# Turning the gathered rows of a mixture-of-experts stage on VectorE and a DMA queue instead of TensorE

## The chip, the cores and the metric

One core of one Trainium2 chip runs the whole program. The metric is the device time of one execution in microseconds (us); lower is better. The engines are TensorE (PE in the rows, its weight loads PEld), VectorE (DVE), ScalarE (ACT), GpSimd (POOL) and SyncE (SP), which here only issues DMAs.

## The reference, cut to what matters

Three stages follow one another: a linear-attention recurrence gives 3072 rows `x` of 384 numbers, a first network (a mixture of 8 experts) sends each row through one expert, and a dense second network follows.

```python
for e in range(E):                       # E = 8, D = 384, F = 1024
    mask = expert_idx == e
    h = np.maximum(x[mask] @ w1[e], 0.0)
    out[mask] = gate_w[mask, None] * (h @ w2[e])
...
h = x @ w_in                             # 3072 x 384 @ 384 x 2048
g = np.maximum(0.01 * h, h)
return (g @ w_out).astype(np.float32)
```

## The kernel before, in words

Each engine has its own instruction stream, and semaphores join them. Every fp32 product is made of three fp32r products (high x high, high x low, low x high parts), so each operand is split by ScalarE (the high part, a copy) and VectorE (the low part, a subtraction).

**The first network** works in 31 windows of 128 slots (`WINDOWS`), sorted by expert. A slot holds a row number, or none. For a window, which the code calls a block while it is ahead, the steps are these:

- POOL gathers its 128 rows from DRAM into `xg[:, u]` (u is the window's parity) by an indirect DMA (`gather`, L763 to L768).
- PE turns them: three 128 x 128 transposes against `ident` into the PSUM bank `gxps` (`turn_gx`, L1738 to L1743; `turn_first` for block 0).
- ACT copies that bank to the high part of `gxT` (`gx_round`, L916), and DVE subtracts to get the low part (`gx_rest`, L1319). `gx_lo` counts the blocks that are ready.
- PE multiplies by w1 (`hidden`, L1761 to L1769): two halves of 9 matmuls each.
- ACT applies ReLU into `hr` (`relu`, L920); DVE turns it in 32 x 32 squares into `hs` (`turn_h`, L1441); SP moves the squares to their places with four DMAs `hds<-hs` (L613); ACT and DVE split them into the parts of `hT` (`h_round` L932, `h_rest` L1448). This path holds from block `FIRST` = 2 on; the first two use PE transposes.
- PE multiplies by w2 (`contract`, L1779 to L1790): 24 matmuls. DVE copies the result to `ys` (`copy_ys`, L1458), POOL scatters it to DRAM.

The stages of different blocks are interleaved by hand. In step `w` PE turns the rows of block w+4, does `hidden` of block w+3 and `contract` of block w. Step 3 (`CLOSE`) does two blocks, 5 and 6. In step w ACT does `gx_round(w+4)`, perhaps a split of a w2, `relu(w+3)`, perhaps a split of a w1, and `h_round(w+1)`. DVE does `gx_rest(w+4)`, the splits' low parts, `turn_h(w+3)`, `h_rest(w+1)` and `copy_ys(w)` in that order. POOL gathers block w+6 and then scatters window w. SP's `move(m)` brings pieces of coming weights (`load_next`, 512 KB each, three for a half) around the four `hds<-hs` DMAs of block m; it waits for `h_turned` and, through `ht_lo`, for `h_rest(m-2)`.

`each_window` writes the first four steps out, makes a loop of the middle ones, and writes out the last `written` steps (5 for DVE, 7 for POOL).

The **second network** follows, whose first products are put among the last three windows; the change doesn't touch it.

Of the kernel before, what the change touches and what calls it, by code (L numbers as in the profile page):

```python
# [16 lines left out]
F32 = mybir.dt.float32  # L17
# [4 lines left out]
ACT = mybir.ActivationFunctionType  # L22
# [3 lines left out]
def build(nc, qka, v, emb, tau, weights, x_dram, y_dram, gate_dram, out):  # L26
    P = 128
# [49 lines left out]
    with ExitStack() as ctx:  # L77
# [113 lines left out]
        with ExitStack() as phase:  # L191
# [19 lines left out]
            idst = sb("idst", [P, 2], I32)  # L211
            yl = sb("yl", [P, 2, GT // SQ, PIECE])
            yf = sb("yf", [P, 2, GT])
            seat(TO_W_IN)
            yT_at = (nc.sbuf_base + 31) // 32 * 32
            yT = sb("yT", [P, 2, 2, KD, GT], F32R)


            hds = nc.alloc_sbuf_tensor_at("hds", [P, 2, F], F32, offset=yT_at)
            hr = nc.alloc_sbuf_tensor_at("hr", [P, 2, HALF], F32, offset=yT_at + 2 * F * 4)  # L220
            assert 3 * F <= 2 * KD * GT
# [4 lines left out]
            hT_odd = nc.alloc_sbuf_tensor_at("hT_odd", [P, 2, F], F32R, offset=os_at)  # L226
            assert 2 * F <= 2 * TG * D
            tokens = sb("tokens", [P, TILES - TG, YW - D])
# [80 lines left out]
        scattered = [sem(f"scattered{j}") for j in range(2)]  # L309
        gx_turned = sem("gx_turned")  # L310
        gx_hi = sem("gx_hi")
        gx_lo = sem("gx_lo")
# [106 lines left out]
        def of(w, u, block):  # L419

            return block % 2 if isinstance(block, int) else 1 - u

        def passed(w, u):
# [82 lines left out]
        def _(sp):  # L506
# [88 lines left out]
            def load_next(due, j):  # L595
                for half, n, flag in due:
# [3 lines left out]
                    with sp.If(flag > 0):  # L600
                        load_piece(sp, half, n, j)

            def move(w, u):

                due = sets_due(w)
                load_next(due, 0)
                sp.wait_ge(h_turned, w * 2 - 2 * FIRST + 2)
                if not (isinstance(w, int) and w < FIRST + 2):  # L610
                    sp.wait_ge(ht_lo, w * 2 - 2)
                for i in range(QUADS):
                    sp.dma_start(hds[:, u, i * QF:(i + 1) * QF], hs[i * SQ:(i + 1) * SQ, u]).then_inc(h_moved[u], 16)  # L613
                load_next(due, 1)
                load_next(due, 2)
# [66 lines left out]
        def _(pool):  # L682
# [81 lines left out]
            def gather(u, rows):  # L764
# [3 lines left out]
                    bounds_check=N - 1, oob_is_err=False).then_inc(gathered[u], 16)  # L768

            gather(0, slot_src[:, 0:1])  # L770
            pool.wait_ge(first_gather_in, 16)
# [10 lines left out]
            def step(w, u):  # L782
                first_gather = w + 5 if isinstance(w, int) and w <= CLOSE else w + 6
                if ahead(w, 6):
                    copied = 3 * w + (1 if isinstance(w, int) and w <= CLOSE else 2)
                    for n in range(2 if isinstance(w, int) and w == CLOSE else 1):
                        at = of(w, 1 - u, first_gather + n)
                        pool.wait_ge(gx_turned, first_gather + n - 1)
                        copy_index(copied + n, isrc, slot_src, first_gather + n, at)
                        gather(at, isrc[:, at:at + 1])  # L790
                    copied = copied + n + 2
                else:
                    copied = WINDOWS - 5 + 2 * (w + 1)
# [35 lines left out]
        def _(act):  # L829
# [86 lines left out]
            def gx_round(w, u):  # L916
                act.wait_ge(gx_turned, w + 1)
                act.activation(gxT[:, u, 0], gxps, ACT.Copy).then_inc(gx_hi, 1)

# [177 lines left out]
        def _(dve):  # L1097
# [219 lines left out]
            after("main")  # L1317
            start("main", dve.tensor_scalar(expert, expert, float(E - 1), None, ALU.min))
            def gx_rest(w, u):  # L1319
                dve.wait_ge(gx_hi, w + 1)  # L1320
                dve.tensor_tensor(gxT[:, u, 1], gxps, gxT[:, u, 0].bitcast(F32), ALU.subtract).then_inc(gx_lo, 1)

# [146 lines left out]
            def step(w, u):  # L1469
# [15 lines left out]
                for block in hidden_blocks(w):  # L1485
# [6 lines left out]
                    if not rows_first(w):  # L1492
                        gx_rest(block + 1, 1 - at)
                    if isinstance(w, int) and block == w + 2:
                        with dve.If(first2 > 0):
                            e2 = dve.snap(e + first1 // (2 * E) + 2)
                            split_lo(dve, e2, next_set(dve, e2), W1_PIECES)
# [18 lines left out]
                if ahead(w, 1) and not (isinstance(w, int) and w == 0):  # L1516
                    for half in range(2):
                        h_rest(w + 1, 1 - u, half)
                if not (isinstance(w, int) and w == 0):
                    copy_ys(w, u)  # L1520
                if ahead(w, 3) and not (isinstance(w, int) and w < CLOSE):
# [15 lines left out]

            each_window(dve, step)

# [34 lines left out]
        def _(pe):  # L1574
# [157 lines left out]
            def turn_first():  # L1732
                pe.wait_ge(gathered[0], 16)
                for k in range(KD):
                    pe.transpose(gx_first[k], xg[:, 0, k * P:(k + 1) * P],
                                 ident[:, :]).then_inc(first_turned if k < KD - 1 else gx_turned, 1)

            def turn_gx(w, u):  # L1738
                pe.wait_ge(gathered[u], w // 2 * 16 + 16 if isinstance(w, int) else w * 8 + (16 - 8 * u))
                pe.wait_ge(gx_lo, w)  # L1740
                for k in range(KD):
                    m = pe.transpose(gxps[:, k * P:(k + 1) * P], xg[:, u, k * P:(k + 1) * P], ident[:, :])  # L1742
                m.then_inc(gx_turned, 1)  # L1743
# [88 lines left out]
            def step(w, u):  # L1832
# [8 lines left out]
                for block, at, block_e in blocks:  # L1841
                    if rows_first(w) and ahead(block, 1):
                        turn_gx(block + 1, 1 - at)
# [131 lines left out]
```

## Time and profile before

| | us |
|---|---|
| median of 3 runs | 801.99 (801.97 to 806.59) |
| the profiled execution | 803.95 |
| its span, first to last instruction | 802.2 |
| PE busy in the span | 791.6 (99%) |
| DVE, ACT, POOL busy | 456.6, 340.6, 207.3 |
| attention and routing | 0 to about 130 |
| first network | about 130 to 410 |
| second network | about 410 to 802 |

The profiled execution is one run; its time holds the span and 1.75 us around it. The granted clock was 0.995 of full speed in the mean.

### The profile page before, as it was taken

How to read it: one execution, taken by the hardware profiler on the slowest of the kernel's cores; microseconds unless marked ns; L12 is line 12 of the kernel's file. 1: busy time of each engine (PE TensorE's matmuls, PEld its weight loads, DVE VectorE, ACT ScalarE, POOL GpSimd, SP SyncE). 2: the span in 40 equal slices, each digit the busy share in tenths (PEclk: the TensorE clock that was granted, in tenths of full speed). 3: DMA queues.
4: the chain of work that ended last, by engine and by line, in shares of the span. 5: the costliest groups of instructions: out<-in, count | busy, mean ns of one | idle time of the engine just before them, and what ended most of it. 6: DMA issues, size and time to landing. Idle time of an engine off the chain costs nothing.

```text
span 802.2 us, 17151 instructions
## 1 busy us (share of the span) xinstructions
PE 791.6 (99%) x5025; PEld 689.1 (86%) x5026; DVE 456.6 (57%) x721; ACT 340.6 (42%) x625; POOL 207.3 (26%) x281
## 2 busy tenths in 40 slices
PE   8999999999999999999999999999999999999998
PEld 7888888889989989989888888888888888888987
DVE  7899987686567476575565343433534433434332
ACT  3554544566446256444344334324323332433323
POOL 6666632223333342331132003001200400100100
PEclk9999998999999999999999999999999999999999
DMA  9997764666774766976640212203202102100301
GB/s 227 273 264 237 223 221 135 237 172 189 259 236 149 245 174 195 288 207 191 155 46 2 39 30 90 39 1 108 50 0 78 40 0 64 55 1 23 96 1 40
DMA packets 74610, 101.84 MB, mean 127 GB/s; under 512 B 35783, under 2 KB 59891, under 8 KB 74560
## 3 DMA queue, kind: packets, MB, share of 16 engines
q1 hardware_dynamic: 65312, 86.13, 37.6%
q0 software_dynamic: 5952, 15.04, 6.1%
q10 hardware_dynamic: 3296, 0.06, 0.2%
q8 instruction: 23, 0.38, 0.2%
q14 instruction: 27, 0.22, 0.1%
HBM read 67.82 MB, written 19.58 MB: 109 GB/s over the span
## 4 chain that ended last, share of the span: by engine, by line
PE 93%; DMA 3%; DVE 1%; issue 1%; POOL 1%; DVEq 0%; ACT 0%; SPq 0%; ACTq 0%; POOLq 0%
PE bank L1813 24%; PE bank L1874 20%; PE bank L1786 16%; PE bank L1766 15%; PE bank L1864 4%; PE bank L1594 3%; PE bank L1632 3%; DMA qkas<-qka 2%; PE bank L1611 2%; PE bank L1640 1%; PE bank L1742 1%; PE bank L1600 1%; PE bank L1585 1%; PE bank L1652 1%; POOL kt L721 0%
## 5 line engine op out<-in xcount | busy, mean ns | idle before, releaser
L1813 PE MATMUL bank<-yT,wts 128*128 128x512 f32 x864 | 204.8, 390 | 0.3 <-DVE g L1368 0.3
L1813 PEld LDWEIGHTS bank<-yT,wts 128*128 128x128 f32 x864 | 161.9, 188 | 34.4 <-DVE g L1368 0.7
L1874 PE MATMUL bank<-gs,wts 128*128 128x512 f32 x720 | 169.7, 389 | 0.0
L1874 PEld LDWEIGHTS bank<-gs,wts 128*128 128x128 f32 x720 | 135.2, 188 | 28.0
L1368 DVE TENSOR_TENSOR g<-bank,small 128x512 f32<-128x512 f32 x96 | 66.0, 687 | 148.8 <-ACT small L975 148.8
L1766 PE MATMUL bank<-wts,gxT 128*128 (+1 forms) x549 | 133.6, 396 | 0.1
L975 ACT ACTIVATE small<-bank 128x512 f32<-128x512 f32 x96 | 57.2, 596 | 166.6 <-PE bank L1813 163.0
L1766 PEld LDWEIGHTS bank<-wts,gxT 128*128 128x128 f32 x549 | 100.8, 188 | 20.8 <-issue 0.7
L1560 DVE TENSOR_TENSOR gs<-g,gs 128x512 fp32r<-128x512 f32 x96 | 66.5, 693 | 66.8 <-ACT gs L1081 66.4
L1081 ACT ACTIVATE gs<-g 128x512 fp32r<-128x512 f32 x96 | 60.8, 633 | 86.0 <-DVE g L1368 84.2
L823 POOL DMA_INDIRECT out<-os,tokens x20 | 19.7, 986 | 291.3 <-ACT os L1070 286.7
L471 DVE TENSOR_TENSOR wts<-raw,wts 128x1024 f32 (+1 forms) x60 | 70.6, 1218 | 7.8 <-ACT wts L465 7.6
L1786 PE MATMUL bank<-wts,hT_even 128*128 x408 | 73.7, 337 | 0.0
L800 POOL DMA_INDIRECT y_rows<-ys,idst x31 | 32.5, 1047 | 156.9 <-DVE ys L1461 156.9
L1786 PEld LDWEIGHTS bank<-wts,hT_even 128*128 128x128 f32 x408 | 71.2, 188 | 1.2
L1446 DVE STREAM_TRANSPOSE hs<-hr 128x512 f32<-128x512 f32 x58 | 39.7, 701 | 45.5 <-ACT hr L929 45.5
L465 ACT ACTIVATE wts<-raw 128x1024 f32 (+1 forms) x60 | 59.8, 1049 | 4.6 <-issue 4.6
L1786 PE MATMUL bank<-wts,hT_odd 128*128 x336 | 60.8, 337 | 0.3 <-issue 0.3
L929 ACT ACTIVATE hr<-bank 128x512 f32<-128x512 f32 x58 | 33.5, 593 | 63.9 <-PE bank L1766 63.9
L1786 PEld LDWEIGHTS bank<-wts,hT_odd 128*128 128x128 f32 x336 | 58.7, 188 | 1.8 <-issue 0.8
L765 POOL DMA_INDIRECT xg<-x_rows,isrc x26 | 29.4, 1131 | 23.1 <-POOL isrc L760 23.1
L716 POOL TENSOR_TENSOR qt<-qkas,decay 112x512 f32<-112x512 f32 x24 | 30.7, 1280 | 16.2 <-DVE decay L1120 14.3
(190 smaller groups left out, 838.4 us busy)
## 6 DMA issues: line engine op xcount, KB each, us to landing
raw<-weights SPq DMA_DIRECT2D x60, 512.0 KB, 4.9
hds<-hs SPq DMA_DIRECT2D x116, 128.0 KB, 3.0
qkas<-qka SPq DMA_DIRECT2D x20, 675.5 KB, 5.7
vs<-v SPq DMA_DIRECT2D x24, 192.0 KB, 4.3
x_rows<-xs SPq DMA_DIRECT2D x24, 192.0 KB, 3.9
yl<-y_rows SPq DMA_DIRECT2D x20, 192.0 KB, 4.3
x_rows<-raw SPq DMA_DIRECT2D x20, 192.0 KB, 3.2
os<-x_rows SPq DMA_DIRECT2D x5, 768.0 KB, 4.5
```

Of the source, the lines that this page charges most:

```text
L465: act.activation(set_of(par, 0, cols), raw[:, cols], ACT.Copy).then_inc(w_hi[j // 3], 1)
L471: dve.tensor_tensor(set_of(par, 1, cols), raw[:, cols], set_of(par, 0, cols).bitcast(F32), ALU.subtract).then_inc(w_lo[j // 3], 1)
L929: act.activation(hr[:, half], hps[u][half][:, :], ACT.Relu).then_inc(relu_done, 1)
L975: act.activation(small[:, f % 2], gps[f % 2][:, :], ACT.Copy, scale=0.01).then_inc(small_done, 1)
L1081: act.activation(gs[:, f % 4, 0], g[:, f % 2], ACT.Copy).then_inc(g_hi, 1)
L1368: dve.tensor_tensor(g[:, f % 2], gps[f % 2][:, :], small[:, f % 2], ALU.max).then_inc(g_done, 1)
L1446: dve.transpose(hs[:, u, half * HALF:(half + 1) * HALF].rearrange("p (n f) -> p n f", f=SQ), hr[:, half].rearrange("p (n f) -> p n f", f=S ...
L1560: dve.tensor_tensor(gs[:, f % 4, 1], g[:, f % 2], gs[:, f % 4, 0].bitcast(F32), ALU.subtract).then_inc(g_lo, 1)
L1766: m = pe.matmul(hps[u][half][:, :], gxT[:, u, x_part, k * P:(k + 1) * P], set_of(par, w_part, slice(n, n + HALF)), start=(k == 0 and (x_pa ...
L1786: m = pe.matmul(yeps[u], ht_of(w, u)[:, h_part, k * P:(k + 1) * P], set_of(par, w_part, slice(n, n + D)), start=(k == 0 and (h_part, w_par ...
L1813: m = pe.matmul(gps[f % 2][:, :], wts[:, 0, w_part, n:n + P], yT[:, 1 - u, y_part, k], start=(k == 0 and (w_part, y_part) == (0, 0)), stop ...
L1874: m = pe.matmul(out_turned[u][k][:, :], wts[:, 1, w_part, n:n + P], gs[:, f % 4, g_part], start=(f == 0 and (w_part, g_part) == (0, 0)), s ...
```

## The change

From block 6 on (`SQUARED`) the gathered rows are no longer turned by PE. DVE turns them in 32 x 32 squares from `xg` into a new tile `xq` (`turn_x`), SP moves the squares with four DMAs into `xd` (`move_x`), and ACT and DVE split `xd` in the place of the PSUM bank. `turn_x(w+6)` stands in DVE's step w between `h_rest(w+1)` and `copy_ys(w)`; `turn_x(8)` stands between the two `turn_h` of step 3. `move_x(m+3)` stands in SP's `move(m)` behind the four `hds<-hs`. `xq` lies in unused room behind `hT_odd`, `xd` on the tile `yf`, which is used only later.

POOL now waits for `x_squared` instead of `gx_turned`, and in the steady state gathers block w+7 in step w, still ahead of the scatter of window w. DVE writes out its last 7 steps.

A transpose in squares puts feature p*3 + k on partition p, where it was k*128 + p. So the PE transposes that stay (blocks 0 to 5) read every third column of `xg`, and w1 is laid out to match on the host, before the launch.

```diff
+            xd = nc.alloc_sbuf_tensor_at("xd", [P, 2, D], F32, offset=yf_at)
...
+            xq = nc.alloc_sbuf_tensor_at("xq", [P, 2, D], F32, offset=os_at + 2 * F * 4)
...
+        SQUARED = 6
+        def x_passed(w, u):
+            return (w * 8 - 8 * (SQUARED - 2) - 8 * u) * QUADS
+        def x_square(ap):
+            return ap.rearrange("p (k i t) -> p k i t", i=QUADS, t=SQ)
+        def x_in_place(u):
+            return xd[:, u].rearrange("p (i k t) -> p k i t", i=QUADS, t=SQ)
+        def squared(w):
+            return not isinstance(w, int) or w >= SQUARED
...
@@ sync @@
+            def move_x(w, u):
+                if not squared(w) or isinstance(w, int) and w >= WINDOWS:
+                    return
+                sp.wait_ge(x_squared, w - SQUARED + 1)
+                for i in range(QUADS):
+                    sp.dma_start(xd[:, u, i * PIECE:(i + 1) * PIECE], xq[i * SQ:(i + 1) * SQ, u]).then_inc(x_moved[u], 16)
...
                     sp.dma_start(hds[:, u, i * QF:(i + 1) * QF], hs[i * SQ:(i + 1) * SQ, u]).then_inc(h_moved[u], 16)
+                move_x(w + 3, 1 - u)
                 load_next(due, 1)
                 load_next(due, 2)
...
@@ gpsimd @@
+            def rows_read(w):
+                if squared(w):
+                    pool.wait_ge(x_squared, w - SQUARED + 1)
+                else:
+                    pool.wait_ge(gx_turned, w + 1)
...
-                first_gather = w + 5 if isinstance(w, int) and w <= CLOSE else w + 6
-                if ahead(w, 6):
-                    copied = 3 * w + (1 if isinstance(w, int) and w <= CLOSE else 2)
-                    for n in range(2 if isinstance(w, int) and w == CLOSE else 1):
-                        at = of(w, 1 - u, first_gather + n)
-                        pool.wait_ge(gx_turned, first_gather + n - 1)
+                sooner = max(0, w - 2) if isinstance(w, int) and w <= CLOSE else 2
+                first_gather = w + 5 + sooner
+                if ahead(w, 7):
+                    copied = 3 * w + 1 + sooner
+                    for n in range(2 if isinstance(w, int) and CLOSE - 1 <= w <= CLOSE else 1):
+                        at = of(w, u, first_gather + n)
+                        rows_read(first_gather + n - 2)
...
@@ scalar @@
             def gx_round(w, u):
-                act.wait_ge(gx_turned, w + 1)
-                act.activation(gxT[:, u, 0], gxps, ACT.Copy).then_inc(gx_hi, 1)
+                if not squared(w):
+                    act.wait_ge(gx_turned, w + 1)
+                    act.activation(gxT[:, u, 0], gxps, ACT.Copy).then_inc(gx_hi, 1)
+                    return
+                act.wait_ge(x_moved[u], x_passed(w, u))
+                act.wait_ge(h_ready, w * 2 - 2)
+                act.activation(x_square(gxT[:, u, 0]), x_in_place(u), ACT.Copy).then_inc(gx_hi, 1)
...
@@ vector @@
+            def turn_x(w, u):
+                dve.wait_ge(gathered[u], w // 2 * 16 + 16 if isinstance(w, int) else w * 8 + (16 - 8 * u))
+                if not (isinstance(w, int) and w < SQUARED + 2):
+                    dve.wait_ge(x_moved[u], x_passed(w, u) - 16 * QUADS)
+                dve.transpose(xq[:, u].rearrange("p (n f) -> p n f", f=SQ),
+                              xg[:, u].rearrange("p (f n) -> p n f", f=SQ)).then_inc(x_squared, 1)
...
+                if squared(w):
+                    dve.tensor_tensor(x_square(gxT[:, u, 1]), x_in_place(u), x_square(gxT[:, u, 0].bitcast(F32)),
+                                      ALU.subtract).then_inc(gx_lo, 1)
...
                         gx_rest(block + 1, 1 - at)
+                    elif isinstance(w, int) and block == CLOSE + 2:
+                        turn_x(block + 3, 1 - at)
...
                 if not (isinstance(w, int) and w == 0):
+                    later = w + 5 if isinstance(w, int) and w < CLOSE else w + 6
+                    if ahead(later, 0):
+                        turn_x(later, of(w, 1 - u, later))
                     copy_ys(w, u)
...
-            each_window(dve, step)
+            each_window(dve, step, 7)
...
@@ tensor @@
-                    m = pe.transpose(gxps[:, k * P:(k + 1) * P], xg[:, u, k * P:(k + 1) * P], ident[:, :])
+                    m = pe.transpose(gxps[:, k * P:(k + 1) * P], xg[:, u, k::KD], ident[:, :])
...
-                    if rows_first(w) and ahead(block, 1):
+                    if rows_first(w) and ahead(block, 1) and not squared(block + 1):
                         turn_gx(block + 1, 1 - at)
```

Three places show how the instructions stand. On PE, at the start of a step in the loop (`L1742` is the transpose of gathered rows, `L1766` and after the change `L1825` the matmuls of `hidden`), before and then after:

```order
L1742 MATMUL bank<-ident,xg 128x128 [waits gx_lo,gathered0]
L1742 MATMUL bank<-ident,xg 128x128 x2
L1824 REGISTER_ALU [waits gx_lo]
L1824 ISA
L1766 REGISTER_ALU [waits relu_done,w1_lo]
L1766 ISA
L1766 MATMUL bank<-wts,gxT 128x512
```

```order
L1883 REGISTER_ALU [waits gx_lo]
L1883 ISA
L1825 REGISTER_ALU [waits relu_done,w1_lo]
L1825 ISA
L1825 MATMUL bank<-wts,gxT 128x512
```

The three transposes and their waits are gone, and the rest stands as it did. On DVE, the end of step 2 and the start of step 3 (`hT_odd` is `h_rest(3)`, `ys` is `copy_ys(2)`, `gxT` is `gx_rest(6)`), before and then after:

```order
L1456 TENSOR_TENSOR hT_odd<-hds,hT_odd 128x512 [waits ht_hi] x2
L1461 COPY ys<-bank 128x384 [waits ye_ready,scattered0]
L442 TENSOR_LOAD wtab
L442 ISA x2
L1321 TENSOR_TENSOR gxT<-bank,gxT 128x384 [waits gx_hi]
```

```order
L1510 TENSOR_TENSOR hT_odd<-hds,hT_odd 128x512 [waits ht_hi] x2
L1366 STREAM_TRANSPOSE xq<-xg 128x384 [waits gathered1]
L1515 COPY ys<-bank 128x384 [waits ye_ready,scattered0]
L464 TENSOR_LOAD wtab
L464 ISA x2
L1372 TENSOR_TENSOR gxT<-xd,gxT 128x384 [waits gx_hi]
```

The transpose of block 7 stands ahead of `ys`, and `gx_rest(6)` reads `xd` in the place of the bank. On SP, the middle of `move(5)` (the `raw` rows are a piece of weights), before and then after:

```order
L613 DMA hds<-hs 128x1x256 [waits ht_lo,h_turned]
L613 DMA hds<-hs 128x1x256 x3
L600 COMPARE_AND_BRANCH
L476 REGISTER_ALU
L476 ISA
L479 ISA [waits w1_lo]
L479 DMA raw<-weights 128x1024
```

```order
L643 DMA hds<-hs 128x1x256 [waits ht_lo,h_turned]
L643 DMA hds<-hs 128x1x256 x3
L631 DMA xd<-xq 128x1x96 [waits x_squared]
L631 DMA xd<-xq 128x1x96 x3
L622 COMPARE_AND_BRANCH
L498 REGISTER_ALU
L498 ISA
L501 ISA [waits w1_lo]
L501 DMA raw<-weights 128x1024
```

Four DMAs and a wait for `x_squared` stand between the squares of the ReLU rows and the pieces of weights.

## Rows read from the trace of the kernel before

**Rows 1.** Chain that ended last, two windows: start us, us, what.
```profile
190.22 4.17 PE bank L1786 x24
194.38 0.33 PE bank L1742 x3
194.71 4.11 PE bank L1766 x18
198.83 4.16 PE bank L1786 x24
```

**Rows 2.** The same view, the last blocks, where nothing is left to turn.
```profile
383.95 4.12 PE bank L1766 x18
388.07 8.33 PE bank L1786 x48
```

**Rows 3.** PE in the transition of steps 2 and 3: start, us, what, [idle before <-releaser].
```profile
170.94 0.49 PE L1742 MATMUL bank<-ident,xg 128*128 128x128 f32 x3
171.18 4.38 PE L1766 MATMUL bank<-wts,gxT 128*128 x18
176.71 0.52 PE L1742 MATMUL bank<-ident,xg 128*128 128x128 f32 x3 [1.15 <-DVE gxT L1321]
177.22 0.95 PE L1766 MATMUL bank<-wts,gxT 128*128 x3
```

**Rows 4.** DVE in time, from step 1's h_rest(2) to step 3's gx_rest(6).
```profile
163.26 1.29 DVE L1456 TENSOR_TENSOR hT_even<-hds,hT_even 128x512 fp32r<-128x512 f32 x2 [1.64 <-ACT hT_even L944]
...
174.34 1.29 DVE L1456 TENSOR_TENSOR hT_odd<-hds,hT_odd 128x512 fp32r<-128x512 f32 x2
175.55 0.55 DVE L1461 COPY ys<-bank 128x384 f32<-128x384 f32 x1
176.01 0.55 DVE L1321 TENSOR_TENSOR gxT<-bank,gxT 128x384 fp32r<-128x384 f32 x1
176.48 1.29 DVE L1446 STREAM_TRANSPOSE hs<-hr 128x512 f32<-128x512 f32 x2
```

**Rows 5.** Who waited for whom, 186 to 384 us: us in total, times, longest.
```profile
ACT gxT L918 <- PE bank L1742: 46.0, 17, 2.8
DVE ys L1461 <- PE bank L1786: 18.9, 12, 1.7
ACT wts L465 <- issue: 4.6, 11, 0.9
```

**Rows 6.** DVE where two splits fall in one step (11).
```profile
249.20 3.50 DVE L471 TENSOR_TENSOR wts<-raw,wts 128x1024 f32 x3 [1.18 <-ACT wts L465]
256.07 1.29 DVE L1456 TENSOR_TENSOR hT_even<-hds,hT_even 128x512 fp32r<-128x512 f32 x2
```

**Rows 7.** PE at that place.
```profile
258.99 4.33 PE L1786 MATMUL bank<-wts,hT_even 128*128 x24
```

**Rows 8.** Busy time of the engines, by stretches: us, PE, PEld, DVE, ACT, POOL, PEclk, DMA share, GB/s.
```profile
186.00:384.00 198.00, 198.00 (x1034) 180.16 (x1034) 126.85 (x177) 98.60 (x154) 64.08 (x111) 1.00 0.70 211
```

**Rows 9.** DMA issues, 186 to 384 us: count, KB each, us to landing.
```profile
raw<-weights SPq DMA_DIRECT2D x39, 512.0 KB, 5.4
hds<-hs SPq DMA_DIRECT2D x93, 128.0 KB, 3.1
```

**Rows 10.** DMA queues over the whole span: packets, MB, share of 16 engines.
```profile
q1 hardware_dynamic: 65312, 86.13, 37.6%
```

**Rows 11.** SP's queue and ACT's splits where a set of weights comes closest.
```profile
324.65 2.53 SPq L613 DMA_DIRECT2D hds<-hs  x4
327.64 2.65 SPq L479 DMA_DIRECT2D raw<-weights  x4
337.64 2.01 ACT L465 ACTIVATE wts<-raw 128x1024 f32 x2 [0.24 <-issue]
...
342.32 2.96 ACT L465 ACTIVATE wts<-raw 128x1024 f32 x3 [0.30 <-issue]
```

**Rows 12.** Weight loads of the transposes, grouped by line: busy us, mean ns, idle before.
```profile
L1742 PEld LDWEIGHTS bank<-ident,xg 128*128 128x128 f32 x90 | 11.5, 140 | 2.8 <-issue 1.5
```

More of the change, by code:

```diff
@@ L212, in build @@
             yl = sb("yl", [P, 2, GT // SQ, PIECE])
+            yf_at = (nc.sbuf_base + 31) // 32 * 32
             yf = sb("yf", [P, 2, GT])
+            assert 2 * D <= 2 * GT
             seat(TO_W_IN)
@@ L226, in build @@
             hT_odd = nc.alloc_sbuf_tensor_at("hT_odd", [P, 2, F], F32R, offset=os_at)
-            assert 2 * F <= 2 * TG * D
+            xq = nc.alloc_sbuf_tensor_at("xq", [P, 2, D], F32, offset=os_at + 2 * F * 4)
+            assert 2 * F + 2 * D <= 2 * TG * D
             tokens = sb("tokens", [P, TILES - TG, YW - D])
@@ L310, in build @@
         gx_turned = sem("gx_turned")
+        x_squared = sem("x_squared")
+        x_moved = [sem(f"x_moved{j}") for j in range(2)]
         gx_hi = sem("gx_hi")
@@ L1318, in _ @@
             start("main", dve.tensor_scalar(expert, expert, float(E - 1), None, ALU.min))
+            def turn_x(w, u):
[4 more added lines that the diff above has]
+                              xg[:, u].rearrange("p (f n) -> p n f", f=SQ)).then_inc(x_squared, 1)
             def gx_rest(w, u):
                 dve.wait_ge(gx_hi, w + 1)
-                dve.tensor_tensor(gxT[:, u, 1], gxps, gxT[:, u, 0].bitcast(F32), ALU.subtract).then_inc(gx_lo, 1)
+                if squared(w):
+                    dve.tensor_tensor(x_square(gxT[:, u, 1]), x_in_place(u), x_square(gxT[:, u, 0].bitcast(F32)),
+                                      ALU.subtract).then_inc(gx_lo, 1)
+                else:
+                    dve.tensor_tensor(gxT[:, u, 1], gxps, gxT[:, u, 0].bitcast(F32), ALU.subtract).then_inc(gx_lo, 1)
             for k in range(KD):
@@ L1734, in turn_first @@
                 for k in range(KD):
-                    pe.transpose(gx_first[k], xg[:, 0, k * P:(k + 1) * P],
+                    pe.transpose(gx_first[k], xg[:, 0, k::KD],
                                  ident[:, :]).then_inc(first_turned if k < KD - 1 else gx_turned, 1)
@@ L1953 @@
     E, D, F = moe_w1.shape
-    w1 = moe_w1[:, features].reshape(E, D // 128, 128, F).transpose(0, 2, 1, 3).reshape(E, 1, 128, -1)
+    w1 = moe_w1[:, features].reshape(E, 1, 128, -1)
     w2 = moe_w2.reshape(E, 4, F // 128, 32, D).transpose(0, 3, 1, 2, 4).reshape(E, 1, 128, -1)
```

## The prediction, made before the change was run

> **What bounds the kernel now.** I read the page first: PE is busy for 791.6 of 802.2 us, so the end is set by what PE does, unless the change makes PE wait. Then the chain that ended last, in order of time. Between 186 and 384 us it is PE alone, in a fixed pattern: 24 matmuls of `contract`, three transposes of gathered rows, 18 matmuls of `hidden` [rows 1]. The reader is to see that the pieces touch: 190.22 + 4.17 = 194.39, + 0.33 = 194.71. The stretches table says the same: PE busy 198.00 of 198.00 us at a granted clock of 1.00, DVE 126.85, ACT 98.60, DMA share 0.70 [rows 8]. A window takes 4.17 + 0.33 + 4.11 = 8.61 us. Where no rows are left to turn, 18 matmuls at 383.95 are followed by `contract` at 388.07, 4.12 us later, and 48 matmuls take 8.33 [rows 2]: a window without transposes takes 4.12 + 4.17 = 8.29. The transposes cost their full 0.33 us on the path; nothing hides them.
>
> The one place before this where PE waits in this stage is at the start: PE waits 1.15 us for DVE's `gx_rest(6)` and goes on at 176.71 [rows 3]. DVE has no idle time from 163.26 to there [rows 4]. So in that stretch DVE is the bound, not PE.
>
> **The change part by part, against the profiled execution's 803.95 us.**
>
> *Removed: PE's transposes of blocks 6 to 30*, 25 turns. At 0.33 us each [rows 1] that is 25 x 0.33 = 8.25 us if all lie on the path. Two don't count. The turn of block 6 at 170.94 stands ahead of the wait for DVE, so what it gives back is waited away again. The turn of block 7 stands right behind that wait, and I count it with the wait, below. 23 turns remain: 23 x 0.33 = 7.6 us.
>
> *Added on DVE: `turn_x`, one per block.* The trace has no transpose of 128 x 384. Two of 128 x 512 take 1.29 us together [rows 4], 0.645 each. By size, 384/512 of that is 0.48; with no saving for the smaller shape it is 0.645. Its source is read with a step of 48 bytes, which no row shows; I keep up to twice 0.52, that is 1.04, as the upper end, and zero can't be had, since the engine must issue it. I take 0.52, near the two contiguous ones. In the steady state this is hidden: DVE is busy 126.85 of 198 us, 5.5 us a window, and becomes 6.0 of 8.29. The cover is gone where weights are split. The tightest is step 11: a w2 and a w1 are split, `h_rest(12)` ends at 256.07 + 1.29 = 257.36, and PE's `contract(12)` needs it at 258.99 [rows 6, 7], 1.6 us later. But `turn_x` stands behind `h_rest` in a step, so what reaches `h_rest` is a delay from the step before, where DVE still waited for PE [rows 5]. What is more, the step begins earlier: ACT today waits for PE's transposes (46.0 us in 17 waits, up to 2.8 [rows 5]) before it may split a w2, and DVE's splits wait 1.18 us for ACT [rows 6]. After the change ACT waits only for `hidden(w+2)`, one `contract` earlier. So DVE comes earlier in the tight steps, and I count nothing there.
>
> At the start DVE is the bound, and there `turn_x(6)` and `turn_x(7)` are both on the path, ahead of `gx_rest(6)`: 2 x 0.52 = 1.04 us. `gx_rest(6)` ends at 176.01 + 0.55 + 1.04 = 177.60, and PE's 18 matmuls of block 6 begin 0.15 later (the distance from 176.56 to 176.71), at 177.75, where they began at 177.22 [rows 3, 4]. Cost 0.53 us, with block 7's turn already settled in it. With 1.04 for each `turn_x` it would be 1.57, with 0.48 it would be 0.45.
>
> *Changed: ACT's and DVE's split of gx read SBUF in the place of a bank.* DVE's 0.55 us for 384 columns from a bank stands beside 1.29 for two of 512 from SBUF [rows 4], 0.645 x 384/512 = 0.48: nothing on the path, and at most 0.1 us either way off it.
>
> *Added on SP: four DMAs and a wait for `x_squared` per block.* Four `hds<-hs` hold SP 2.53 us and land 3.1 us after issue [rows 9, 11]. In `move(m)` the wait for `x_squared` of block m+3 comes behind a wait for `h_rest(m-2)`, and `turn_x(m+3)` follows that at once on DVE, so SP loses under a microsecond to the wait; then the issue, about 2.5 us. SP's queue per window: 2.5 + 2.5 + 39 pieces x 0.66 / 23 = 1.1, some 6.1 of 8.29. The x rows are there some 0.5 + 2.5 + 3.1 = 6 us after `h_rest(w+1)` of step w; `hidden(w+6)` begins two windows later, 16 us. Behind the wait stand pieces of weights, on which more below. DMA engines: in this stretch they are busy 0.70 x 8.61 = 6.0 us a window. The new packets are 512 a window of 384 bytes. The mean packet of this queue has 86.13 MB / 65312 = 1319 bytes and takes 0.376 x 16 x 802.2 us / 65312 = 74 ns [rows 10]. By bytes a new one takes 22 ns (0.7 us a window over 16 engines), at the full mean 74 ns (2.4 us). The share becomes 0.81 to 1.02. I take 40 ns, 1.3 us, a share of 0.88, since smaller packets are rarely free but this is nearer to the byte end. No cost on the path.
>
> *POOL* gathers a block earlier, after the scatter of the step before: rows of block w+7 are asked for about two windows ahead of `turn_x(w+7)`. Nothing. If POOL's gather were late, DVE would stop in `turn_x`, and `copy_ys` stands behind it.
>
> *PE's transposes that stay* (18 for blocks 0 to 5) read every third column, 12 bytes apart, in the weight load of 140 ns [rows 12]. Contiguous today; bounds 0 and, at twice the load, 18 x 0.14 = 2.5 us. Loads overlap the matmul before; I take 0.1.
>
> The Trainium skill's page "SBUF — State Buffer", section "Door 1: The DMA port swizzle (why `[64,N]` ≈ `[32,N]`)", speaks against the last points: SBUF has lines of 16 bytes, at least two reads must fall in a line for full speed, and each move to a new line costs. At 12 bytes a line gets 1.33 reads, at 48 bytes each read is in a line of its own, so by the rule both new reads are slower. No row here has such a stride. It is the second rival.
>
> Sum: -7.6 + 0.53 + 0.1 = -7.0. 803.95 becomes 797.0; carried to the median of 801.99 (2 us lower than the profiled run) it is 795.0 us.
>
> **The rivals.**
>
> *Weights come late.* In the set that comes closest, four pieces are issued at 327.64 to 330.3, 5.4 us to landing, longer in a queue; ACT takes the first at 338.6 and the last near 344.3 [rows 9, 11]. The x DMAs push these issues back by 2.5 us, engines that are busy 0.88 stretch them by perhaps 2, and by then PE runs 5 us ahead of today's times, which moves both ends alike. For it: little slack, 3 to 8 us. Against: ACT never waits for a DMA today, only for issue [rows 5], and a late piece has 1.6 to 2.8 us before PE feels it. If three sets are late by about 1.2 us net, 3.5 of the 7.0 are lost: 798.5.
>
> *Strided reads are slow.* `turn_x` at 1.04 costs the start another 1.04, and the 18 loads half their upper bound, 1.25: 795.0 + 2.3 = 797.3. The 16-byte lines of the page named above would be the reason.
>
> *Everything is given back.* If DVE at the start catches up elsewhere (by ACT's earlier split of w2, or because `turn_x(6)` falls in slack) all 25 turns count: 8.25, 793.7. For it: ACT's 46 us of waits go. Against: DVE's row of work has no gap from 163.26 on.
>
> *Slower: the DMA engines become the bound.* The point is where the new packets take more than 8.61 - 6.0 = 2.6 us a window, 81 ns each. At 90 ns they take 2.9, a window is 8.9, and 23 windows cost 23 x 0.29 = 6.7 instead of giving 7.6: 801.99 + 6.7 + 0.6 = 809.3. For it: the share is 0.70 already, and a weight set comes in bursts. Against: the mean of 74 ns belongs to packets of 1319 bytes.
>
> **How the numbers follow.** The forecast, PE still the bound and 7.0 us gained, 0.54; weights late 0.17; strides slow 0.11; all of it given back 0.14; DMA the bound 0.04. A measurement of this kernel tells about 1% (8.0 us) from no change. Faster by over 1% means under 794.0: the fourth case and a little of the first, 0.15. Slower by over 1% (over 810.0) is part of the last: 0.02. The rest, 0.83, lies within 1%, though mostly on the faster side. The range reaches from 793.3 (all 25 turns and 0.4 us more) to 799.0 (weights late in three places, with a little on top).
>
> **What the profile would show.** Right: in the chain, `hidden` follows `contract` with no piece between and a window lasts 8.29; 15 PE transposes of xg remain in `turn_gx`; `turn_x` takes some 0.57 us by its row; block 6's `hidden` begins about half a microsecond later against the end of block 5's; ACT's waits for PE's transposes are gone from block 6 on; the DMA share from 186 us is near 0.88. Wrong: waits of PE for `wts` or `gxT` behind 186 us (weights or x late), a `turn_x` of 1 us, weight loads of the 18 transposes well over 140 ns, or ACT waiting for `xd` long enough that ReLU falls behind PE.

## The result, and the profile after

| | before | after |
|---|---|---|
| median, us | 802.34 | 824.61 (823.84 to 828.23) |
| span of the profiled execution, us | 802.2 | 822.4 |
| PE busy in the span | 791.6 (99%) | 791.6 (96%) |

The ratio is 1.0276, with a 95% interval of 1.0256 to 1.0296. The change costs 22 us where I had forecast a gain of 7, and over 810 us I had given a chance of 0.02. PE is busy for as long as before, though 25 turns of it are gone, and 20 us more of the span are not PE's.

The first reading is by windows. PE starts `contract` of one block after another; these are the starts in both traces, counted from the first instruction, in us (the first matmul of each group; "step" is the distance to the start of the block before).

Some of the blocks:

```
block    before  step     after  step
 2       166.77          165.50
 3       181.43 14.66    183.11 17.61
 4       190.06  8.63    191.40  8.29
 8       224.52          224.91  8.29
 9       233.13  8.61    236.21 11.30
12       258.99  8.63    268.35 13.90
13       267.60  8.61    279.31 10.96
22       345.16  8.63    358.89 10.85
23       353.76  8.61    372.67 13.77
27       387.91          408.17
```

Ten of the 24 steps from block 3 to block 27 take 8.29 to 8.35 us: the transposes are gone and a window takes the 8.29 us that I had worked out. All 24 would take 24 x 8.29 = 199.0 us. They take 408.17 - 183.11 = 225.1, so 26.1 us are lost in the others. The sum: -7.5 for the turns (206.5 became 199.0), +2.95 at the start (17.61 against 14.66) and +26.1 make 21.5 us. Block 2 began 1.3 us earlier than in the kernel before, and from block 27 to the end both take the same to 0.1 us; that gives the 20.2 us between the two spans. I don't put the 1.3 us down to the change: in the traces of this document, which do much the same up to there, block 2 begins anywhere from 164.3 to 169.7 us.

What ended the waits, in the changed kernel from 186 to 410 us (us in total, times, longest):

```profile
POOL y_rows L838 <- DVE ys L1515: 138.4, 21, 13.6
ACT gxT L961 <- DMA xd<-xq: 91.4, 19, 8.6
DVE gxT L1372 <- ACT gxT L961: 44.5, 14, 6.7
PE bank L1845 <- DVE hT_even L1510: 8.1, 5, 4.2
```

ACT's waits for a transpose of PE [rows 5] are gone as forecast, and in their place stand waits of up to 8.6 us for the moved rows `xd`. PE itself now waits for `h_rest`. The same stretch by busy time (us, PE, PEld, DVE, ACT, POOL, PEclk, DMA share, GB/s), against [rows 8]:

```profile
186.00:410.00 224.00, 207.65 (x1004) 184.51 (x1003) 144.62 (x203) 101.11 (x158) 64.61 (x112) 0.97 0.72 213
```

No engine and no DMA queue is full: DVE 0.65, DMA 0.72, and PE is idle for 16.35 us. What is late is seen on SP. Its own waits, same stretch, the kernel before (to 384 us):

```profile
SPq L611 <- DVE hT_even L1456: 27.2, 7, 6.3
SPq L611 <- DVE hT_odd L1456: 18.3, 7, 5.8
SPq L479 <- DVE wts L471: 0.8, 1, 0.8
```

and the changed one (to 410 us):

```profile
SPq L643 <- DVE hs L1500: 2.5, 5, 0.5
SPq L641 <- DVE hT_even L1510: 1.8, 3, 1.0
SPq L641 <- DVE hT_odd L1510: 1.1, 1, 1.1
```

46 us of slack became 5. SP hardly waits for anybody any more: it is behind. The view of SP in time shows it, for the place of the loss at block 9:

```profile
218.12 1.10 SPq L501 DMA_DIRECT2D raw<-weights  x2
221.30 2.63 SPq L643 DMA_DIRECT2D hds<-hs  x4
223.98 2.56 SPq L631 DMA_DIRECT2D xd<-xq  x4
229.63 2.52 SPq L643 DMA_DIRECT2D hds<-hs  x4
232.27 2.59 SPq L631 DMA_DIRECT2D xd<-xq  x4
```

and who pays, DVE, ACT and PE:

```profile
211.17 0.87 DVE L1366 STREAM_TRANSPOSE xq<-xg 128x384 f32<-128x384 f32 x1
...
230.57 3.50 DVE L493 TENSOR_TENSOR wts<-raw,wts 128x1024 f32 x3 [1.38 <-issue]
234.00 1.29 DVE L1500 STREAM_TRANSPOSE hs<-hr 128x512 f32<-128x512 f32 x2
235.22 1.25 DVE L1510 TENSOR_TENSOR hT_odd<-hds,hT_odd 128x512 fp32r<-128x512 f32 x2
```
```profile
228.07 0.52 ACT L961 ACTIVATE gxT<-xd 128x384 fp32r<-128x384 f32 x1 [2.30 <-DMA xd<-xq]
229.17 2.96 ACT L487 ACTIVATE wts<-raw 128x1024 f32 x3 [0.57 <-issue]
```
```profile
236.21 5.99 PE L1845 MATMUL bank<-wts,hT_odd 128*128 x24 [2.13 <-DVE hT_odd L1510]
242.04 4.28 PE L1825 MATMUL bank<-wts,gxT 128*128 x18
```

DVE turned x(12) at 211.17. SP came to issue it at 223.98, 12.8 us later, because it works through its stream in order. ACT could begin to round it at 228.07, when it had landed. ACT rounds x ahead of the split of a w2, so that split began at 229.17; DVE's half of it, the squares and `h_rest(9)` followed, and PE began `contract(9)` 2.13 us late. Then the 24 matmuls took 5.99 us instead of 4.33.

That last step is the clock. The granted clock around it (columns as above):

```profile
228.00:234.00 6.00, 5.51 (x26) 4.23 (x24) 3.99 (x5) 5.36 (x8) 1.81 (x5) 1.00 0.53 153
234.00:236.00 2.00, 0.08 (x1) 0.00 (x0) 2.00 (x5) 0.13 (x1) 0.00 (x0) 1.00 0.43 101
236.00:239.00 3.00, 2.79 (x9) 2.79 (x10) 3.00 (x6) 2.21 (x5) 0.41 (x1) 0.57 0.24 31
239.00:242.00 3.00, 3.00 (x16) 3.00 (x16) 2.34 (x4) 0.43 (x1) 2.10 (x4) 0.86 0.94 355
242.00:250.00 8.00, 8.00 (x43) 7.26 (x42) 1.95 (x4) 2.12 (x5) 2.84 (x7) 1.00 0.92 274
```

PE stood still in 234 to 236, and behind that it ran partly at the lower of its two levels (1.2 of 2.4 GHz), at 0.57 and 0.86 of full speed. A wait of 2.13 us cost 1.66 us more in the matmuls behind it. The waits of 4.21 and 2.64 us at blocks 12 and 23 were followed by 7.00 and 5.97 us where 4.33 and 4.28 are usual. In these three places alone the lower clock took 6.0 of the 26.1 us; PE's idle time of 186 to 410 us is 16.35 of them, and the other 9.8 are PE busy for longer than 24 windows of 8.29 need.

**Where SP's time goes.** The views count only the DMA issues. The trace also holds SP's register, branch and table-load instructions. From the `hds` issue of block 8 to that of block 28, per window in us:

```
                        before  after  x by one DMA  half by POOL
issues hds<-hs            2.44   2.58      2.49          2.59
issues xd<-xq                -   2.44      0.62          1.27
issues raw<-weights       0.65   0.58      0.53          0.63
table loads of wtab       0.65   0.54      0.72          0.57
a window, all together    8.59   9.51      8.61          8.80
```

A window in which no piece of weights is brought can be read whole: from the first table load at 257.10 to the next at 265.30, 8.20 us. Its eight issues hold 5.1 us with the gaps between them (some 0.64 each), two table loads with what unpacks them, from 257.10 to 258.33, hold 1.2, and the conditionals of `load_next` and what belongs to them the remaining 1.9, though nothing was brought. The 35 pieces of the 20 windows, at some 0.6 us each, bring that to 9.25, and some issues take longer than 0.6 us (up to 1.97); the mean is 9.5 us, and the window of the other engines is 8.29. That is **theory A**: SP's stream of instructions is the bound. **Theory B** is the transfers themselves (bytes, packets), **theory C** VectorE's `turn_x` and the wait for it.

### The profile page after: what moved, and what is told of

It is laid out like the page before. It is cut to its first block, busy times and chain, and to the rows that moved or that the text cites. A ratio compares the mean times of both kernels' runs of the same rounds, so it can differ in the third digit from the quotient of the medians.

```text
span 822.4 us, 17148 instructions
## 1 busy us (share of the span) xinstructions
PE 791.6 (96%) x4950; PEld 684.2 (83%) x4951; DVE 474.4 (58%) x746; ACT 340.8 (41%) x625; POOL 210.2 (26%) x281
## 3 DMA queue, kind: packets, MB, share of 16 engines
q1 hardware_dynamic: 79712, 91.05, 38.9%
## 4 chain that ended last, share of the span: by engine, by line
PE 71%; SPq 9%; issue 6%; DMA 5%; DVE 3%; ACT 2%; ACTq 1%; DVEq 1%; POOL 1%; POOLq 0%
PE bank L1872 24%; PE bank L1933 20%; PE bank L1845 7%; PE bank L1825 5%; PE bank L1923 4%; SPq L643 3%; SPq L631 3%; PE bank L1653 3%; PE bank L1691 2%; DMA qkas<-qka 2%; PE bank L1670 2%; DMA xd<-xq 2%; PE bank L1699 1%; PE bank L1659 1%; ACT wts L487 1%
## 5 line engine op out<-in xcount | busy, mean ns | idle before, releaser
L1933 PE MATMUL bank<-gs,wts 128*128 128x512 f32 x720 | 169.7, 389 | 0.0
L1825 PE MATMUL bank<-wts,gxT 128*128 (+1 forms) x549 | 135.6, 401 | 8.7 <-DVE gxT L1372 7.4
L1825 PEld LDWEIGHTS bank<-wts,gxT 128*128 128x128 f32 x549 | 104.1, 192 | 33.2 <-issue 12.6
L1845 PE MATMUL bank<-wts,hT_even 128*128 x408 | 76.8, 346 | 8.1 <-DVE hT_even L1510 8.1
L1845 PEld LDWEIGHTS bank<-wts,hT_even 128*128 128x128 f32 x408 | 73.4, 194 | 10.9 <-issue 10.2
L1845 PE MATMUL bank<-wts,hT_odd 128*128 x336 | 62.6, 343 | 3.1 <-DVE hT_odd L1510 2.9
L961 ACT ACTIVATE gxT<-xd 128x384 fp32r<-128x384 f32 x25 | 13.1, 524 | 102.9 <-DMA xd<-xq 97.0
L1372 DVE TENSOR_TENSOR gxT<-xd,gxT 128x384 fp32r<-128x384 f32 x25 | 14.0, 559 | 49.9 <-ACT gxT L961 46.7
```

Of the source, the lines that this page charges most:

```text
L1825: m = pe.matmul(hps[u][half][:, :], gxT[:, u, x_part, k * P:(k + 1) * P], set_of(par, w_part, slice(n, n + HALF)), start=(k == 0 and (x_pa ...
L1845: m = pe.matmul(yeps[u], ht_of(w, u)[:, h_part, k * P:(k + 1) * P], set_of(par, w_part, slice(n, n + D)), start=(k == 0 and (h_part, w_par ...
L1933: m = pe.matmul(out_turned[u][k][:, :], wts[:, 1, w_part, n:n + P], gs[:, f % 4, g_part], start=(f == 0 and (w_part, g_part) == (0, 0)), s ...
```

## The experiments

**The four DMAs without the rest of the change**, in the kernel before (to all but the first and last blocks):

```diff
+  sp.wait_ge(spare_in[u], ...)      # the spare DMAs of two blocks before
+  for i in range(QUADS):
+      sp.dma_start(spare[:, u, i * PIECE:(i + 1) * PIECE],
+                   weights[0, 0, i * SQ:(i + 1) * SQ, 0:D]).then_inc(spare_in[u], 16)
```

> The kernel before, with four more DMAs of 48 KB per block on SyncE behind the ReLU rows' DMAs, from a constant array in DRAM into an unused tile; nothing reads it and nothing else changes. Theory A (SyncE's issue is the bound): SyncE needs 9.5 us a window where a window takes 8.6, so it falls behind by 0.9 us a window, 22 us over 25 windows, of which the ReLU rows' slack of some 10 us hides a part: 808 to 822 us. Theory B (bytes on the DMA engines): also slower, with SyncE waiting as before. Theory C (VectorE's transposes, the x chain): unchanged, 801 to 804.

816.12 us against 803.18, ratio 1.0142 (1.0099 to 1.0185). SP's period rises from 8.59 to 9.46 us. There is no `turn_x`, no other engine waits for these transfers, and PE keeps its transposes: C is not needed for the loss. From 186 to 400 us SP waits for nobody at all, where B had it wait as before. That speaks for A; this run alone doesn't rule B out.

**One DMA for four**, and **four tiny ones**, in the changed kernel:

```diff
-  for i in range(QUADS):
-      sp.dma_start(xd[:, u, i * PIECE:(i + 1) * PIECE], xq[i * SQ:(i + 1) * SQ, u])
+  sp.dma_start(xd[:, u], xq[:, u])
```

(and the waits count one DMA in the place of four). The placing of the squares is left out.

> The changed kernel, but the rows turned in squares are moved by one DMA of 192 KB per block in place of four of 48 KB. The placing of the squares is left out (the same bytes go straight across); all waits stay. Theory A, SyncE's own instruction stream is the bound (2.5 us for the four ReLU DMAs, 2.55 for the four x DMAs, 3.1 of table loads and branches, and weight pieces: 9.5 us a window): three issues of 0.6 us fewer make it 7.7 us, under PE's 8.29, and the time falls to 797 to 804 us. Theory B, the DMA engines are too busy with the bytes: stays at 820 to 825. Theory C, VectorE's slow transposes (0.87 us) or the wait for x_squared on SyncE: stays at 820 to 825.

803.97 us in one run, against 802.25. The same 192 KB a block with three issues fewer give back 20.6 us. SP waits again, 26.1 us from 186 to 384. Each partition's row goes as one run here, so there are fewer packets too, 3600 more than in the kernel before where the changed one has 14400 more; that rival is taken up below.

```diff
+  for i in range(QUADS):
+      sp.dma_start(xd[:, u, i * PIECE:i * PIECE + 1], xq[i * SQ:(i + 1) * SQ, u, 0:QUADS])
```

Most of x is left out here.

> The changed kernel with four x DMAs per block as before, but each moves 128 elements of 4 bytes in place of 128 runs of 384 bytes (most of x is left out of the move). Theory A (SyncE's issue): four issues of 0.6 us remain, 818 to 825 us. Theory B (bytes on the DMA engines): 796 to 804. Theory C (VectorE): 820 to 825.

825.39 us in one run, 0.4 over A's range. A 96th of the bytes, and the time stays. The busy time of 186 to 410 us shows the bytes gone from the DMA share, 0.72 to 0.66, and nothing else changed:

```profile
186.00:410.00 224.00, 208.43 (x1008) 185.70 (x1008) 145.67 (x204) 100.62 (x158) 64.38 (x112) 0.97 0.66 194
```

B falls as to the bytes, and as to the time of the DMA engines: their share is under the 0.70 of the kernel before. The number of packets is left, 14400 more here as in the changed kernel. The kernels with one DMA, with half by POOL (8800 more) and with all by POOL (3200 more) have fewer issues on SP and fewer packets at once, so they can't tell the two apart. The runs with fewer conditionals and with x by ScalarE have all 14400, and they can.

**Two of the four issued by POOL** (with a semaphore of their own):

```diff
-  for i in range(QUADS):
+  for i in range(2):
       sp.dma_start(xd[:, u, ...], xq[...])
+  for i in range(2, QUADS):      # POOL, ahead of the next gather
+      pool.dma_start(xd[:, u, ...], xq[...]).then_inc(x_pooled[u], 16)
```

(in outline; ACT and DVE wait for both semaphores).

> The changed kernel with two of the four x DMAs on SyncE and two on POOL: the same transfers, the same order of waits. Theory A (SyncE's stream: 9.51 us a window in blocks 8 to 28 of the changed kernel, no wait left in it): 2 x 0.65 us less is 8.2 us, just under the 8.29 us window, so nearly all of the loss goes: 805 to 809 us, and SyncE's waits for h_rest come back. Rival (the waits added on SyncE, or the transfers themselves): 815 to 825 us.

808.13 us against 802.95, ratio 1.0073 (1.0053 to 1.0092): inside A's range. SP waits again, 17 us from 186 to 384:

```profile
SPq L642 <- DVE hT_even L1523: 9.5, 4, 3.5
SPq L642 <- DVE hT_odd L1523: 6.0, 3, 4.1
SPq L632 <- DVE xq L1379: 1.6, 3, 0.6
```

So four, two, one and none of these issues on SP (the last is the POOL kernel below) give 824.6, 808.1, 804.0 and 804.2 us. With two, SP's stream without its waits is 8.80 - 17.1/22.5 = 8.0 us, under the window of 8.29. The loss is there as long as SP's own stream is longer than the window, and most of it is gone once it isn't.

**Fewer conditionals**, the second and third piece of a half under one:

```diff
-  load_next(due, 1)
-  load_next(due, 2)
+  load_next(due, [1, 2])
```

(in outline; `load_next` brings both pieces under its one conditional).

> The changed kernel, where SyncE's second and third piece of a weight half are issued under one conditional instead of two, so that a window has one to two conditionals fewer and the same DMAs. Theory A (SyncE's stream of issues, loads and branches takes 9.5 us of an 8.29 us window): 0.5 to 1 us a window less on SyncE, over 22 windows 10 to 18 us: 807 to 815 us. Rival (the four DMA issues alone, or the landing of the transfers, set it and the branches are free): 823 to 826 us.

821.60 us (ratio 1.0231, 1.0212 to 1.0251). A miss of A's number: in the 20 windows counted, SP's conditional branches fell from 126 to 86, two a window, but SP's period only from 9.51 to 9.33 us. A branch costs some 0.09 us here, not the 0.25 to 0.5 that I had assumed. The direction and the order agree with A (0.18 us x 22 windows = 4.0, measured 3.0, with the two intervals apart), and the rival's 823 to 826 is missed as well. DMAs, bytes and packets are the same here as in the changed kernel; only SP's stream is shorter, and the time falls. The control stream isn't free, but its weight lies in the table loads and in the issues.

**x issued by ScalarE**, two DMAs ahead of each ReLU:

```diff
+  if rows_first(w):
+      move_x(block + 2, at, range(2 * half, 2 * half + 2))    # act.dma_start
   relu(block, at, half)
```

(in outline).

> The changed kernel with the four x DMAs issued by ScalarE, two before each half's ReLU, in place of SyncE; same bytes and packets. Theory A: SyncE is back at some 7 us a window, ScalarE takes 2.2 us a window more (it is busy 4.4 of 8.3): 797 to 804 us, 2 to 3 us worse than that if ScalarE's issues delay ReLU where weights are split. Theory B (DMA engines): 818 to 825. Theory C: 818 to 825.

815.38 us, ratio 1.0171 (1.0142 to 1.0201): under what B and C had, but over A's number too (up to 807 with the ReLU delayed). SP is relieved: with all 14400 packets still there it waits 48.8 us from 186 to 400, and 9 us come back. So the packets aren't what holds SP up. But the 2.5 us of issues now stand ahead of ACT's ReLUs. ACT's waits, 186 to 400 us:

```profile
ACT hr L970 <- issue: 47.7, 28, 4.3
ACT gxT L952 <- DMA xd<-xq: 39.7, 16, 4.6
```

The issues cost ACT about what they cost SP (0.62 us each). That ACT has no room for them where PE waits for the ReLU's path is my reading of these waits; no run tests it by itself.

**x issued by POOL**, behind its wait for `x_squared` and ahead of the next gather:

```diff
   rows_read(first_gather + n - 2)
+  if squared(first_gather + n - 2):
+      move_x(first_gather + n - 2, at)      # pool.dma_start
```

(in outline).

> The changed kernel with the four x DMAs issued by GpSimd, ahead of its next gather, where it waits for x_squared anyway. Theory A: 797 to 804 us if GpSimd's four issues of about 1 us each leave its scatter in time; if they don't, the second network's first rows come late or copy_ys waits, 805 to 812. Theory B and C: 818 to 825.

804.17 us (10 runs, 801.53 to 805.72), ratio 1.0019 (1.0005 to 1.0032). 20 us come back, with the same bytes as in the changed kernel, and SP waits 42.7 us from 186 to 384. But the 7 that the removed turns should give don't come. The start takes 15.87 us, and windows 8 to 13 (all but 11) and 22 to 24 take 8.8 to 10.0. ACT is still late there:

```profile
336.21 0.53 ACT L962 ACTIVATE gxT<-xd 128x384 fp32r<-128x384 f32 x1 [8.49 <-DMA xd<-xq]
337.85 1.09 ACT L973 ACTIVATE hr<-bank 128x512 f32<-128x512 f32 x2 [1.11 <-issue]
338.86 2.01 ACT L487 ACTIVATE wts<-raw 128x1024 f32 x2
```
```profile
327.30 1.06 POOL L839 DMA_INDIRECT y_rows<-ys,idst  x1 [1.97 <-DVE ys L1516]
328.36 2.24 POOL L795 DMA_DIRECT2D xd<-xq  x4
```

x(25) was turned at 325.07 but issued at 328.36, behind a scatter, while SP issued four pieces of weights from 328.85 on, and it landed at 336.2, 5.6 us after its last issue. Three runs, all built on this kernel, tried to tell what of this costs. **Theory P**: `turn_x` on VectorE. **Theory Q**: ACT's rounding of a late x stands ahead of the ReLU.

```diff
-  xg[:, u].rearrange("p (f n) -> p n f", f=SQ)
+  xg[:, u].rearrange("p (n f) -> p n f", f=SQ)
```

The features then stand in another order than w1's rows; putting them right is left out.

> The kernel with x issued by POOL, where turn_x reads the gathered row contiguously instead of with a stride of 12 elements; the features of blocks 6 to 30 then stand in another order than W1's rows, and nothing else is changed. The open question is why the POOL kernel (804.2 us) does not reach the 795 us that 23 removed turns should give. Theory P (VectorE: turn_x at 0.87 us delays the stretch between contraction 2 and 3, 15.87 us there against 14.66 before, and the later windows): turn_x falls to some 0.5 us, the stretch to about 15.2 us, the time to 801 to 803. Theory Q (ScalarE: gx_round stands ahead of the ReLUs and waits for x, 93 us of waits in 21 windows, so that a late x delays ReLU, squares and the next activation): turn_x gets shorter by the same amount but x arrives at most 0.4 us sooner, so the time stays at 803 to 805.

803.80 us (1.0010, 0.9999 to 1.0021), not to be told from 804.17. The price of the stride is now measured, `turn_x` before and here (min/median/max ns):

```profile
L1366 DVE STREAM_TRANSPOSE xq<-xg x25: 830/871/903, 163.2 to 384.3; 128x384 f32<-128x384 f32 x25
```
```profile
L1367 DVE STREAM_TRANSPOSE xq<-xg x25: 532/569/578, 164.7 to 370.4; 128x384 f32<-128x384 f32 x25
```

and the start took 15.39 in place of 15.87 us. P had 801 to 803 us and accounts for half a microsecond at most.

```diff
-  SQUARED = 6
+  SQUARED = 8
```

> The kernel with x issued by POOL, but blocks 6 and 7 turned by TensorE as before; squares from block 8 on. P: the stretch from contraction 2 to 3 goes back from 15.87 to about 14.7 us, for 2 x 0.33 us of turns: 803 us or a little less. Q: windows 8 to 13 and 22 to 24 still lose 0.5 to 1.7 us each; the time stays within 1 us of 804.

804.79 us (1.0023, 1.0009 to 1.0037). The start is 14.61 us as forecast, but in the profiled run blocks 8 and 22 lost 2.1 and 3.6 us and ate it up. That run was the slowest of the ten (808.66), so its windows don't explain the median.

```diff
   for half in range(2):
       relu(block, at, half)
+  gx_round(block + 1, 1 - at)       # was ahead of the ReLUs; gx_rest likewise behind turn_h
```

(in outline, with squares from block 8 on as in the last one).

> As the last one, and the rounding of x(block + 1) stands behind the two ReLUs of the block on ScalarE, its rest behind the block's squares on VectorE. Q: late x no longer delays the ReLU; windows 4 to 26 all take 8.29 to 8.35 us, which gives back up to 5 us: 797 to 799.5 us. P: no different from the last one (803). If TensorE now waits for the rest of x, it shows as a wait of hidden (bank<-wts,gxT) for gxT, and the time is over 804.

806.74 us (1.0045, 1.0028 to 1.0062), against 804.79 for the kernel that it is built on: no better, so Q as I put it falls. PE, one of the four such places of the profiled run (814.02, the slowest of five):

```profile
327.21 5.99 PE L1826 MATMUL bank<-wts,gxT 128*128 x18 [1.80 <-DVE gxT L1373]
```

The rest of x then stands behind DVE's 4.6 us of weight splits and comes too late for `hidden`. Moving the reader back doesn't help; x must come earlier.

**x issued ahead of the scatter**: POOL moves x(w+6) in step w, as soon as it is turned, and only then waits for `ys`. The edit is shown in outline. The first kernel squares from block 6, the second from block 8.

```diff
   copy_index(copied, idst, slot_dst, w, u)
+  rows_read(w + 6)
+  move_x(w + 6, u)
   pool.wait_ge(ys_ready, w + 1)
```

> The kernel with x issued by POOL, but POOL moves x(w + 6) ahead of the scatter of window w, right after VectorE has turned it, where it moved x(w + 5) behind the next wait for ys. In the kernel before this one x(25) was issued 3.3 us after turn_x(25) and stood behind four weight pieces in the DMA queues (landed 5.6 us after its last issue, 336.2), and ScalarE's rounding, ReLU and weight split all came late behind it. Theory Q' (the late x in windows that also load weights costs the windows of over 8.29 us): x is there two windows ahead, ScalarE's 93 us of waits for x go, windows 8 to 13 and 22 to 24 come down to some 8.4 us: 797 to 800 us. Rival R (VectorE's own work in the windows with weights, now 0.87 us more, makes them long): 803 to 805 us, with VectorE busy through those windows.

> The same with blocks 6 and 7 turned by TensorE. By either theory the stretch from contraction 2 to 3 is 1.2 us shorter and two windows 0.33 us longer: 0.5 us less than the kernel before this one, so 796.5 to 799.5 by Q', 802.5 to 804.5 by R.

**798.90 us** (798.20 to 799.59), ratio to before 0.9956 (0.9941 to 0.9971), against 802.95 on the same chip. This version beats both kernels, by 0.44% against the one before. PE and the others, 186 to 384 us:

```profile
186.00:384.00 198.00, 197.78 (x999) 178.95 (x997) 145.40 (x203) 101.14 (x158) 121.20 (x202) 1.00 0.78 237
```

All windows from 4 to 27 take 8.29 to 8.48 us but one of 8.77. Over 24 windows, 6.5 us are gained (206.5 became 199.9), and the start gives 2.9 of them back (17.54 against 14.66); that is 3.7 us, against 4.05 between the medians. VectorE does as much as in the kernels before it (145.4 us), so rival R falls. ACT still waits for x, but 52.0 us from 186 to 384 where it was 81.2, and at most 5.7 us at a time where it was 9.5. SP's slack is back, 38 us for `h_rest` from 186 to 384 (46 in the kernel before). The one from block 8 gave 800.48 (0.9972, 0.9958 to 0.9986), 1.6 us more where both theories had it 0.5 less. Its profiled run has the short start, 14.59 us, and loses 2.2 us at blocks 22 to 24 (9.63, 9.07, 8.37). It was the fastest of its twelve (797.98), so it can't show where the median loses. The two intervals overlap; why the start's gain isn't kept stays open.

## Why the prediction was wrong

**The step that failed** is "SP's queue per window: 2.5 + 2.5 + 39 pieces x 0.66/23 = 1.1, some 6.1 of 8.29". I counted the DMA issues as if they were all that SP executes. The trace has 9.51 us a window: the issues are 5.6 of it (my 6.1 holds the gaps within them), and 3.9 are table loads, register arithmetic, conditionals and all the gaps between instructions, none of which the page counts as busy. So the next step failed too, that x is there "some 0.5 + 2.5 + 3.1 = 6 us after `h_rest(w+1)`": x(12) was there 16.8 us after `h_rest(7)`, 12.8 of them before SP issued it. The kernel before could have told me: its SP waited only 46.3 us in 198, about 2.0 a window of 8.61, so its stream held 6.6 without x. Adding 4 x 0.65 = 2.6 gives 9.2, over the new window of 8.29. The slack was to be read from SP's waits, not from the issues' busy time. Of the signs that I had named for a wrong forecast, two came: ACT waits for `xd`, and PE waits for `gxT` behind 186 us.

**None of the four rivals** was this mechanism. The slower one was at the DMA engines. Their share was forecast at 0.88 and is 0.72 (0.78 in the kernel that runs at 8.3 us a window). From the queue's rows, 0.389 x 16 x 822.4 - 0.376 x 16 x 802.2 = 292 us for 79712 - 65312 = 14400 packets more, 20 ns each: the byte end of my bounds, not the 40 that I took. The rival "weights come late" named the right kind of place, SP's pushed-back issues, but looked only at the 2.5 us of one window and not at a queue that falls behind in each.

**Right: what is removed.** Undisturbed windows take 8.29 us, and the kernel with x on time shows it in nearly all. On its chip the forecast's gain of 7.0 would be 795.9 us; it has 798.9, and 2.3 of the 3.0 missing are the start.

**Mis-sized: `turn_x`.** 0.871 us, not 0.52, inside the bounds; contiguous it is 0.569, so the size was near and the stride costs 0.30. The Trainium skill's page "SBUF — State Buffer", section "Door 1: The DMA port swizzle (why `[64,N]` ≈ `[32,N]`)", says that each access that crosses to a new 16-byte line pays a penalty; the trace agrees for DVE's 48 bytes (871 against 569 ns) and for PE's weight loads at 12 bytes, 140 ns in [rows 12] and now:

```profile
L1801 PEld LDWEIGHTS bank<-ident,xg x15: 188/194/202, 134.5 to 161.2; 128*128 128x128 f32 x15
```

The 54 ns each (1.0 us for 18, inside my bounds) didn't reach the path: blocks 0 to 2 are 9.59 and 8.61 us apart in both kernels.

**Mis-sized: the start.** `gx_rest(6)` ends 176.67 - 165.50 = 11.17 us after the start of `contract(2)`, where it was 176.56 - 166.77 = 9.79, and `hidden(6)` begins at 11.79 against 10.45: 1.34 us instead of 0.53. `gx_rest(6)` is 1.38 us later, not 1.04: the two `turn_x` took 0.68 more than I had put, of which half was made good elsewhere. And PE began 0.62 us behind it, not the 0.15 that I took from a transpose:

```profile
177.29 5.98 PE L1825 MATMUL bank<-wts,gxT 128*128 x18 [3.22 <-DVE gxT L1372]
```

The wait is 3.22 us where it was 1.15 [rows 3], and the granted clock falls behind it (0.73 in 177 to 180, 0.77 in 180 to 184), and from there to `contract(3)` it takes 5.82 us in the place of 4.21: that is the other 1.6 us of the 2.95.

## What to carry to other kernels

Before DMAs are added to an engine's stream, read how long that engine waits per period; that is all the room it has, and branches, table loads and gaps have used the rest though no row counts them as busy. Each of these SBUF-to-SBUF DMAs cost its issuer about 0.65 us, with 0.5, 48 or 192 KB, so fewer DMAs, or another issuer that itself has slack, was worth more here than smaller ones. Put an issue ahead of waits that it doesn't need: the same four DMAs on POOL gave 804.2 us behind the scatter and 798.9 ahead of it (1.0019 and 0.9956 of the kernel before, intervals apart).

## What the runs showed of the hardware

- One issue of x on SP holds it for the same time with 48 KB and with 0.5 KB (0.60 us, 0.65 with the gap; 2.44 and 2.43 us a window for four), and one of 192 KB for 0.62. It isn't the same for every DMA: a piece of weights of 512 KB from DRAM holds SP for 0.33 us. POOL issues four of x in 2.24 us, and the same four copies make 128 packets from its queue, where they make 576 from SP's (3200 and 14400 for 25 blocks). The Trainium skill's page "DMA: Bandwidth & Descriptors", section "Issuing engines are not separate DMA queues", says that spreading DMAs over engines saves only the sequencer's time to start them, usually small beside the transfer. In this trace the transfer is longer than its issue too (0.60 us against some 4 from SP's issue of x(12) to ACT's start on it), and still the time on the sequencer was the bound: 16.5 us came back when two of four moved to POOL.
- A wait of PE of 2 to 4 us is mostly followed by a stretch at the lower clock that costs another 1.7 to 2.7 us, so that a late operand costs 1.5 to 1.8 times its lateness (2.13 + 1.66, 4.21 + 2.67, 2.64 + 1.69, 3.22 + 1.70 us in the changed kernel). Not always: at the start the POOL kernel waited 3.09 us and went on at a granted clock of 1.00, where the one that issues ahead of the scatter waited 3.10 us and went on at 0.79 and 0.65. The kernel with the ReLU first has waits of 2.00 and 2.41 us with 18 matmuls in 4.36 and 4.37 us behind them. What decides between the cases I don't know.
- A DMA of 48 KB that is issued beside four weight pieces of 512 KB landed 5.6 us after its issue, though it came from another engine's queue.
